# Splitting the output weights of a rational layer on the scalar and vector engines, and a nested polynomial read from PSUM

## The chip, the cores and the metric

One NeuronCore of a Trainium2 chip runs the whole program. The metric is the device time of one launch in microseconds; the program runs on one core, so that core's time is the time. Below, PE is the tensor engine, DVE the vector engine, ACT the scalar engine, POOL the GpSimd engine and SP the engine that issues the DMAs here.

## The reference

Three layers run one after the other. The change touches the second.

```python
# 1: attention restricted by clusters: q, k, v of 2 x 8 heads, 768 tokens, 64 dims
# 2: the rational layer: x [1536, 512], w_in [512, 2048], w_out [2048, 512]
h = x @ w_in
h2 = h * h
h3 = h2 * h
P = a[0] + a[1] * h + a[2] * h2 + a[3] * h3
Q = 1.0 + np.abs(b[0]) * np.abs(h) + np.abs(b[1]) * h2
g = P / (Q + 1e-06)
return (g @ w_out).astype(np.float32)
# 3: eight experts [512 -> 1024 -> 512] mixed with Sinkhorn weights
```

## The kernel before, in words

**Precision.** Every matmul operand is split into a high part (the value rounded to the format that PE takes) and a low part (the rest), and each product is the sum of three matmuls: high by high, high by low, low by high. Weights must therefore be split after they are loaded: first the high part, then the low part, which needs the high one.

**The rational layer.** The 1536 tokens are 4 chunks of 384 (HS), the 2048 hidden columns are 16 blocks of 128 (f). One chunk and one block are a unit u = 16 c + f, so there are 64 units. PE computes the hidden values of a unit with 12 matmuls of 128x384 into PSUM bank f % 4 (function hidden, L501 to L503) and its share of the output with 12 more (function mlp_out, L582 to L584). mlp_chunk writes PE's order out by hand: hidden of unit u + 4, then the output of unit u. mlp_out of unit u waits for the low part of its g (semaphore g_lo) and, whatever the chunk, for the low part of weight block f (wout_lo).

**What ACT does in step u** (mlp_step in the scalar block): mlp_reads(u), four activations that read PSUM: the square into TA (L790), the scaled absolute value into TB (L791), a3 h + a2 into TC (L792), a1 h + a0 into TD (L794); then mlp_recip(u - 1), a logarithm and an exponential that give an approximate reciprocal of Q (L800, L802); then g_hi_part(u - 2), the high part of g (L807).

**What DVE does in step u** (mlp_step in the vector block), eight instructions: the Q sum of unit u (L1018), the first Newton product of unit u - 1 (L1025, which waits for the exponential of L802), TC times TA (L1028), Q plus 1 (L1030), the second Newton step of u - 1 (L1033), the addition of TD (L1037), the low part of g of unit u - 2 (gl, L1041), and g of unit u - 1 (L1046). Both engines take their instructions strictly in the order written.

**The output weights.** w_out comes in 16 blocks of 128x512, called pieces here. SP loads them (load_wout, L364) into wst_out, which has two places: piece f may be loaded once the low part of piece f - 2 has been made, because that frees its place. POOL makes the high and the low part of all 16 (L1268, and L1204 by the helper lo_part called at L1270) in a loop that starts when attention's last product is done (pv_done). These lines order the loads:

```python
at_least(sp, wout_lo, fp * 2 + r - 1)
sp.dma_start(wst_out[:, r, :], tile.rearrange("p a d -> p (a d)")).then_inc(wout_in[r], 16)
```

**Around it.** In the last steps of attention ACT copies the last rows of x (L770), POOL makes their low part, and the first four hidden units are put in between. Late in the rational layer, after unit 58's hidden values, POOL splits the first expert weights (L1297, L1298, L1328 and L1204).

Of the kernel before, what the change touches and what calls it, by code (L numbers as in the profile page):

```python
# [18 lines left out]
F32 = mybir.dt.float32  # L19
F32R = mybir.dt.float32r  # L20
ALU = mybir.AluOpType
ACT = mybir.ActivationFunctionType
# [4 lines left out]
P = 128  # L27
B, H, S, D = 2, 8, 768, 64
NC = 16
BH = B * H  # L30
QT = S // P
HS = S // 2
# [11 lines left out]
AHEAD = 4  # L44
SINK = 8
SCALE = 1.0 / 8.0
PENALTY = -(2.0 ** 100)
OHW = 112


def at_least(eng, sem, value):

    if isinstance(value, int) and value <= 0:
        return
    eng.wait_ge(sem, value)


def build(nc, qT, kT, v, cent, ident_d, desc_d, fold_d, w_in, w_out, a_d, b_d, w_gate, w1, w2, out):
    with ExitStack() as ctx:
# [11 lines left out]
        def sem(name):  # L71
            return ctx.enter_context(nc.semaphore(name))

        def pack(start, *specs):

            got = []
            for name, shape, dt in specs:
                got.append(sb(name, start, shape, dt))
                start += (size(*shape[1:]) + 31) // 32 * 32
            return got, start  # L80
# [1 line left out]

        (XTh, XTl, ab, babs, wgf, fold), o_win = pack(
            0, ("XTh", [P, B, DT, S], F32R), ("XTl", [P, B, DT, S], F32R),
            ("ab", [P, 4], F32), ("babs", [P, 2], F32), ("wgf", [P, DT, E], F32),
            ("fold", [P, E], F32))
        (winh, winl), o_free = pack(o_win, ("winh", [P, FT, DT, P], F32R), ("winl", [P, FT, DT, P], F32R))

# [14 lines left out]
        centn = xt[:, 3 * D:4 * D]  # L103


        (wouth, woutl, TA, TB, TC, TD, gh, gl, wst_out), o2 = pack(
            o_free,
            ("wouth", [P, FT, DM], F32R), ("woutl", [P, FT, DM], F32R),
            ("TA", [P, 4, HS], F32), ("TB", [P, 4, HS], F32), ("TC", [P, 4, HS], F32), ("TD", [P, 2, HS], F32),
            ("gh", [P, 2, HS], F32R), ("gl", [P, 2, HS], F32R), ("wst_out", [P, 2, DM], F32))  # L110


# [60 lines left out]
        wout_in = (sem("wout_in0"), sem("wout_in1"))  # L173
        wout_hi, wout_lo = sem("wout_hi"), sem("wout_lo")
        hid_done, hid_read = sem("hid_done"), sem("hid_read")
        q_part, q_done = sem("q_part"), sem("q_done")
        num_done = sem("num_done")
        recip0 = sem("recip0")
        ln_done = sem("ln_done")
        newton1, q_raw = sem("newton1"), sem("q_raw")  # L180
        newton_r, num_step = sem("newton_r"), sem("num_step")
        g_done, g_hi, g_lo = sem("g_done"), sem("g_hi"), sem("g_lo")
        mlp_done = sem("mlp_done")
        x2_hi, x2_lo = sem("x2_hi"), sem("x2_lo")
# [505 lines left out]
        def _(act):  # L690
# [88 lines left out]
                part(p, 0, 0)  # L779
            values_hi(0, 0)  # L780
            act.wait_ge(const_in, 16 * NCONST)
            act.activation(babs[:], bwork[:, 0:2], ACT.Abs).then_inc(coef_ready, 1)


            def mlp_reads(c, f):
                u = c * FT + f
                act.wait_ge(hid_done, u + 1)
                at_least(act, g_lo, u - 3)
                h = ps[:, f % 4, 0:HS]
                act.activation(TA[:, f % 4, :], h, ACT.Square)  # L790
                act.activation(TB[:, f % 4, :], h, ACT.Abs, scale=babs[:, 0:1]).then_inc(q_part, 1)  # L791
                act.activation(TC[:, f % 4, :], h, ACT.Identity, scale=ab[:, 3:4], bias=ab[:, 2:3])  # L792
                at_least(act, num_done, u - 1)
                act.activation(TD[:, f % 2, :], h, ACT.Identity, scale=ab[:, 1:2],  # L794
                               bias=ab[:, 0:1]).then_inc(hid_read, 1)

            def mlp_recip(u, f):

                act.wait_ge(q_done, u + 1)
                act.activation(TA[:, f % 4, :], TB[:, f % 4, :], ACT.Ln).then_inc(ln_done, 1)  # L800
                act.wait_ge(ln_done, u + 1)
                act.activation(TA[:, f % 4, :], TA[:, f % 4, :], ACT.Exp, scale=-1.0).then_inc(recip0, 1)  # L802

            def g_hi_part(u, f):
                act.wait_ge(g_done, u + 1)
                at_least(act, mlp_done, u - 1)
                act.activation(gh[:, f % 2, :], TC[:, f % 4, :], ACT.Copy).then_inc(g_hi, 1)  # L807

            def x2_hi_part(c):

# [4 lines left out]
            def mlp_step(c, f, reads=True):  # L815
                u = c * FT + f
                first = isinstance(c, int) and c == 0
                if reads:
                    mlp_reads(c, f)
                if f == 3 and not first:  # L820
                    x2_hi_part(c - 1)
                if (f >= 1 or not first) and not (isinstance(c, int) and u > NCH * FT):
                    mlp_recip(u - 1, (f - 1) % FT)
                if f >= 2 or not first:
                    g_hi_part(u - 2, (f - 2) % FT)

            def first_reads(t):
                if t == 1:
                    act.wait_ge(coef_ready, 1)
                    mlp_reads(0, 0)  # L830

            steps(emit, first_reads)(act)
            for f in range(1, FT):
# [74 lines left out]
        def _(dve):  # L908
# [98 lines left out]
                                      ALU.add).then_inc(x_done, 1)  # L1007


            def mlp_step(c, f, reads=True):  # L1010
                u = c * FT + f
                first = isinstance(c, int) and c == 0
                s, s1, s2 = f % 4, (f - 1) % 4, (f - 2) % 4
                one = (f >= 1 or not first) and not (isinstance(c, int) and u > NCH * FT)
                two = f >= 2 or not first
                if reads:
                    dve.wait_ge(q_part, u + 1)
                    dve.scalar_tensor_tensor(out=TB[:, s, :], in0=TA[:, s, :], scalar=babs[:, 1:2], in1=TB[:, s, :],  # L1018
                                             op0=ALU.mult, op1=ALU.add).then_inc(q_raw, 1)
                if f == 3 and not first:  # L1020
                    x2_lo_part(c - 1)
                if one:
                    dve.wait_ge(recip0, u)

                    dve.tensor_tensor(TB[:, s1, :], TB[:, s1, :], TA[:, s1, :], ALU.mult).then_inc(newton1, 1)  # L1025
                if reads:
                    dve.wait_ge(hid_read, u + 1)
                    dve.tensor_tensor(TC[:, s, :], TC[:, s, :], TA[:, s, :], ALU.mult).then_inc(num_step, 1)  # L1028
                    dve.wait_ge(q_raw, u + 1)
                    dve.tensor_scalar(TB[:, s, :], TB[:, s, :], 1.0, 1e-6, ALU.add, ALU.add).then_inc(q_done, 1)  # L1030
                if one:
                    dve.wait_ge(newton1, u)
                    dve.scalar_tensor_tensor(out=TA[:, s1, :], in0=TB[:, s1, :], scalar=2.0, in1=TA[:, s1, :],  # L1033
                                             op0=ALU.subtract, op1=ALU.mult).then_inc(newton_r, 1)
                if reads:
                    dve.wait_ge(num_step, u + 1)
                    dve.tensor_tensor(TC[:, s, :], TC[:, s, :], TD[:, f % 2, :], ALU.add).then_inc(num_done, 1)  # L1037
                if two:
                    dve.wait_ge(g_hi, u - 1)
                    at_least(dve, mlp_done, u - 3)  # L1040
                    dve.tensor_tensor(gl[:, f % 2, :], TC[:, s2, :], gh[:, f % 2, :].bitcast(F32),  # L1041
                                      ALU.subtract).then_inc(g_lo, 1)
                if one:
                    dve.wait_ge(newton_r, u)
                    dve.wait_ge(num_done, u)
                    dve.scalar_tensor_tensor(out=TC[:, s1, :], in0=TC[:, s1, :], scalar=-1.0, in1=TA[:, s1, :],  # L1046
                                             op0=ALU.mult, op1=ALU.mult).then_inc(g_done, 1)

            def x2_lo_part(c):
                for d in range(DT):  # L1050
# [8 lines left out]
            def first_step(t):  # L1059
                if t == 1:  # L1060
                    mlp_step(0, 0)

            steps(emit, first_step)(dve)
            for f in range(1, FT):
                mlp_step(0, f)
            with dve.Fori(1, NCH) as c:
                for f in range(FT):
                    mlp_step(c, f)
# [125 lines left out]
        def _(pool):  # L1194
            pool.memset(OH[:], 0.0).then_inc(zero_ready, 1)

            def carry_wait():


                pool.sem_inc(waits_carried, 1)  # L1200

            def lo_part(dst, x, hi):

                return pool.tensor_tensor(dst, x, hi.bitcast(F32), ALU.subtract)  # L1204
# [52 lines left out]
                part(p, 0, 0)  # L1257
            steps(emit)(pool)


            pool.wait_ge(pv_done, 2 * BH)
            with pool.Fori(0, FT // 2) as fp:
                for r in range(2):
                    f = fp * 2 + r
                    fh, fl = (x[:].rearrange("p f d -> p (f d)")[:, bass.ds(f * DM, DM)] for x in (wouth, woutl))
                    pool.wait_ge(wout_in[r], (fp + 1) * 16)
                    carry_wait()
                    pool.tensor_copy(fh, wst_out[:, r, :]).then_inc(wout_hi, 1)  # L1268
                    pool.wait_ge(wout_hi, f + 1)
                    lo_part(fl, wst_out[:, r, :], fh).then_inc(wout_lo, 1)  # L1270


            def add(dst, x, y):

                return pool.tensor_tensor(dst, x, y, ALU.add)
# [152 lines left out]
```

## Time and profile before

| | |
|---|---|
| device time, median of 3 runs | 1678.51 us (1678.4 to 1681.99) |
| the profiled execution: its own time | 1679.58 us |
| the profiled execution: span from first to last instruction | 1677.7 us |
| PE busy | 1575.9 us, 94% |
| PE weight loads busy | 1438.6 us, 86% |
| DVE busy | 1136.7 us, 68% |
| ACT busy | 649.1 us, 39% |
| POOL busy | 673.0 us, 40% |

The whole program's shares are an average over three layers with different limits. The rational layer lies from about 335 us to 642 us of the span (first matmul of L501 to last matmul of L584). A timeline gives each instruction's start, its length and, in brackets, how long its engine had been idle and what released it; a following instruction of the same engine can start a little before the end of the one ahead.

### The profile page before, as it was taken

The numbers are of one execution on the slowest core, as the hardware profiler recorded it, in microseconds if no ns is written. First come the engines' busy times: TensorE is split into PE (matmuls) and PEld (weight loads), VectorE is DVE, ScalarE is ACT, GpSimd is POOL, SyncE is SP. The second block draws the span as 40 slices with busy tenths as digits, with TensorE's granted clock in tenths as the row PEclk, the third lists the DMA queues.
The fourth block names the chain that finished last, engine by engine and source line by source line (L and its number), as shares of the span: only waits on it lengthen the run. The fifth ranks groups of instructions, "written<-read, shape, count | busy, mean of one in ns | idle before, by whom it ended". The sixth has DMA issues, their size and how long they took to land.

```text
span 1677.7 us, 25909 instructions
## 1 busy us (share of the span) xinstructions
PE 1575.9 (94%) x8265; PEld 1438.6 (86%) x8265; DVE 1136.7 (68%) x2133; ACT 649.1 (39%) x1348; POOL 673.0 (40%) x516
## 2 busy tenths in 40 slices
PE   5888888869999998699999999999999999999998
PEld 5777777769999998598998998998998998988987
DVE  5889898889989992534656555555655565565555
ACT  5888788856888871012111111111111111111111
POOL 4767676571000020268543344244244344334230
PEclk9999999989999998799999999999999999999999
DMA  4322232120000010010110110110110111011001
GB/s 110 89 78 84 82 88 82 31 70 19 1 1 0 13 38 13 26 38 14 38 51 13 39 51 13 38 50 16 47 38 31 32 38 38 25 38 38 25 13 75
DMA packets 76404, 67.92 MB, mean 40 GB/s; under 512 B 17345, under 2 KB 58433, under 8 KB 76353
## 3 DMA queue, kind: packets, MB, share of 16 engines
q1 hardware_dynamic: 76352, 67.25, 13.6%
q8 instruction: 30, 0.49, 0.1%
q14 instruction: 22, 0.17, 0.0%
HBM read 64.09 MB, written 3.15 MB: 40 GB/s over the span
## 4 chain that ended last, share of the span: by engine, by line
PE 78%; DVE 11%; issue 5%; ACT 4%; POOL 0%; DVEq 0%; ACTq 0%; DMA 0%; POOLq 0%
PE ps L657 10%; PE ps L658 10%; PE ps L659 10%; PE ps L546 8%; PE ps L545 8%; PE ps L547 8%; PE ps L582 2%; PE ps L583 2%; PE ps L584 2%; PE ps L501 2%; PE ps L503 2%; PE ps L502 2%; DVE OH L952 2%; PE ps L522 1%; PE ps L477 1%
## 5 line engine op out<-in xcount | busy, mean ns | idle before, releaser
L1160 DVE SCALAR_TENSOR_TENSOR acc<-ps,gate,acc 128x512 f32<-128x512 f32 x372 | 278.9, 750 | 191.5 <-PE ps L659 191.5
L657 PE MATMUL ps<-w2h,hh 128*128 128x512 f32 x768 | 300.9, 392 | 13.0 <-DVE acc L1157 9.6
L658 PE MATMUL ps<-w2l,hh 128*128 128x512 f32 x768 | 300.7, 392 | 0.0
L659 PE MATMUL ps<-w2h,hl 128*128 128x512 f32 x768 | 300.4, 391 | 0.0
L854 ACT ACTIVATE hh<-ps 128x384 fp32r<-128x384 f32 x256 | 119.4, 491 | 401.5 <-PE ps L547 210.8
L1123 DVE SCALAR_TENSOR_TENSOR hl<-ps,hh 128x384 fp32r<-128x384 f32 x256 | 141.3, 553 | 113.3 <-ACT hh L854 107.5
L890 ACT ACTIVATE p1s<-ps 128x384 f32<-128x384 f32 x56 | 27.5, 491 | 453.8 <-PE ps L547 453.8
L657 PEld LDWEIGHTS ps<-w2h,hh 128*128 128x128 f32 x768 | 145.0, 189 | 42.4 <-DVE acc L1157 10.1
L659 PEld LDWEIGHTS ps<-w2h,hl 128*128 128x128 f32 x768 | 145.2, 189 | 30.6
L658 PEld LDWEIGHTS ps<-w2l,hh 128*128 128x128 f32 x768 | 145.1, 189 | 28.2
L1316 POOL TENSOR_SCALAR w1h<-raw 128x1792 fp32r<-128x1792 f32 x28 | 47.8, 1707 | 292.3 <-PE ps L547 291.9
L547 PE MATMUL ps<-XTh,w1l 128*128 128x384 f32 x448 | 150.8, 337 | 0.0
L546 PE MATMUL ps<-XTl,w1h 128*128 128x384 f32 x448 | 150.8, 337 | 0.0
L545 PE MATMUL ps<-XTh,w1h 128*128 128x384 f32 x448 | 150.7, 336 | 0.0
L1241 POOL TENSOR_SCALAR Pb<-Pb,small 128x768 f32<-128x768 f32 x96 | 87.2, 908 | 99.0 <-DVE small L979 98.2
L1204 POOL TENSOR_TENSOR w1l<-raw,w1h 128x1792 fp32r<-128x1792 f32 (+2 forms) x36 | 124.2, 3455 | 2.7
L546 PE MATMUL ps<-tl,w1h 128*128 128x384 f32 x336 | 113.5, 338 | 0.0
L545 PE MATMUL ps<-th,w1h 128*128 128x384 f32 x336 | 112.9, 336 | 0.0
L547 PE MATMUL ps<-th,w1l 128*128 128x384 f32 x336 | 112.6, 335 | 0.0
L477 PE MATMUL ps<-ident,Pb 128*128 128x128 f32 x576 | 95.5, 293 | 15.6 <-DVE PTl L994 10.6
L582 PE MATMUL ps<-gh,wouth 128*128 128x384 f32 x256 | 88.5, 346 | 22.0 <-DVE gl L1041 21.9
L1297 POOL TENSOR_SCALAR w1h<-raw 128x768 fp32r<-128x768 f32 x4 | 3.7, 929 | 262.3 <-PE ps L503 209.2
(147 smaller groups left out, 3771.8 us busy)
## 6 DMA issues: line engine op xcount, KB each, us to landing
raw<-in_w SPq DMA_DIRECT2D x64, 256.0 KB, 3.1
raw<-in_w SPq DMA_DIRECT2D x32, 512.0 KB, 3.3
qd<-in_qT SPq DMA_DIRECT2D x32, 192.0 KB, 3.2
kd<-in_kT SPq DMA_DIRECT2D x32, 192.0 KB, 3.1
wst_in<-in_w_in SPq DMA_DIRECT2D x16, 256.0 KB, 2.7
wst_out<-in_w_out SPq DMA_DIRECT2D x16, 256.0 KB, 2.6
qk<-in_qT SPq DMA_DIRECT2D x16, 192.0 KB, 3.1
qk<-in_kT SPq DMA_DIRECT2D x16, 192.0 KB, 3.3
```

The costliest lines, as they stand in the source:

```text
L477: last = pe.transpose(ps[:, 4 + a, k * P:(k + 1) * P], Pb[:, t1 % 2, a, k * P:(k + 1) * P], ident[:])
L545: pe.matmul(o, ah, xh[:, k, :], start=(start and k == 0), stop=False, skip_group_check=True)
L546: pe.matmul(o, ah, xl[:, k, :], start=False, stop=False, skip_group_check=True)
L547: last = pe.matmul(o, al, xh[:, k, :], start=False, stop=(k == 1), skip_group_check=True)
L582: pe.matmul(o, wouth[:, f, ds_], gh[:, f % 2, :], start=(f == 0), stop=False)
L657: pe.matmul(o, lh, w2h[b][:, fh, :], start=(fh == 0), stop=False)
L658: pe.matmul(o, lh, w2l[b][:, fh, :], start=False, stop=False)
L659: last = pe.matmul(o, ll, w2h[b][:, fh, :], start=False, stop=(fh == 1))
L854: act.activation(hh[hbuf(e, s)][:, fh, thalf, :], ps[:, bank, 0:HS], ACT.Relu).then_inc(h_hi, 1)
L1123: dve.scalar_tensor_tensor(out=hl[hb][:, fh, thalf, :], in0=ps[:, q, 0:HS], scalar=0.0, in1=hh[hb][:, fh, thalf, :].bitcast(F32), op0=ALU.max,
L1160: dve.scalar_tensor_tensor(out=acc[:, tt, :], in0=y, scalar=g, in1=acc[:, tt, :], op0=ALU.mult, op1=ALU.add).then_inc(y_added, 1)
L1204: return pool.tensor_tensor(dst, x, hi.bitcast(F32), ALU.subtract)
```

## The change

The splitting of w_out leaves POOL. In the first chunk (c = 0) ACT makes the high part of piece f in its step f, right behind mlp_reads and ahead of mlp_recip of the unit before; DVE makes the low part of piece f - 1 at the end of its step f. Piece 0's high part is made by ACT in the tail of attention, and the reciprocal of unit 0 now comes ahead of the reads of unit 1. The DMAs and their waits stay as they are.

The polynomial is evaluated by nesting: ((a3 h + a2) h + a1) h + a0, the two products reading h from PSUM on DVE, so TD and its activation go, and the constant a0 is added in the instruction that multiplies by the reciprocal. The 1 + 1e-6 of Q is folded into the logarithm's bias and into the first Newton product, so the addition of L1030 goes. The sign that L1046 used to turn is turned in the two instructions that make the high and low part of g.

```diff
+Q_ONE = 1.0 + 1e-6
...
-        (wouth, woutl, TA, TB, TC, TD, gh, gl, wst_out), o2 = pack(
+        (wouth, woutl, TA, TB, TC, gh, gl, wst_out), o2 = pack(
...
+            def wout_piece_hi(f):
+
+                if f == 0:
+                    act.wait_ge(pv_done, 2 * BH)
+                act.wait_ge(wout_in[f % 2], 16 * (f // 2 + 1))
+                act.activation(wouth[:, f, :], wst_out[:, f % 2, :], ACT.Copy).then_inc(wout_hi, 1)
...
-                act.activation(TC[:, f % 4, :], h, ACT.Identity, scale=ab[:, 3:4], bias=ab[:, 2:3])
-                at_least(act, num_done, u - 1)
-                act.activation(TD[:, f % 2, :], h, ACT.Identity, scale=ab[:, 1:2],
-                               bias=ab[:, 0:1]).then_inc(hid_read, 1)
+                act.activation(TC[:, f % 4, :], h, ACT.Identity, scale=ab[:, 3:4],
+                               bias=ab[:, 2:3]).then_inc(hid_scaled, 1)
...
-                act.activation(TA[:, f % 4, :], TB[:, f % 4, :], ACT.Ln).then_inc(ln_done, 1)
+                act.activation(TA[:, f % 4, :], TB[:, f % 4, :], ACT.Ln, bias=babs[:, 2:3]).then_inc(ln_done, 1)
...
                 first = isinstance(c, int) and c == 0
+                if first and f == 1:
+                    mlp_recip(0, 0)
                 if reads:
                     mlp_reads(c, f)
+                if first:
+                    wout_piece_hi(f)
                 if f == 3 and not first:
                     x2_hi_part(c - 1)
-                if (f >= 1 or not first) and not (isinstance(c, int) and u > NCH * FT):
+                if (f >= 2 or not first) and not (isinstance(c, int) and u > NCH * FT):
                     mlp_recip(u - 1, (f - 1) % FT)
...
+                if t == QT - 1:
+                    wout_piece_hi(0)
...
+            def wout_piece_lo(f):
+
+                dve.wait_ge(wout_hi, f + 1)
...
+                dve.tensor_tensor(woutl[:, f, :], wst_out[:, f % 2, :], wouth[:, f, :].bitcast(F32),
+                                  ALU.subtract).then_inc(wout_lo, 1)
...
-                    dve.tensor_tensor(TB[:, s1, :], TB[:, s1, :], TA[:, s1, :], ALU.mult).then_inc(newton1, 1)
+                    dve.scalar_tensor_tensor(out=TB[:, s1, :], in0=TB[:, s1, :], scalar=Q_ONE, in1=TA[:, s1, :],
+                                             op0=ALU.add, op1=ALU.mult).then_inc(newton1, 1)
                 if reads:
-                    dve.wait_ge(hid_read, u + 1)
-                    dve.tensor_tensor(TC[:, s, :], TC[:, s, :], TA[:, s, :], ALU.mult).then_inc(num_step, 1)
-                    dve.wait_ge(q_raw, u + 1)
-                    dve.tensor_scalar(TB[:, s, :], TB[:, s, :], 1.0, 1e-6, ALU.add, ALU.add).then_inc(q_done, 1)
+                    dve.wait_ge(hid_scaled, u + 1)
+                    dve.tensor_tensor(TC[:, s, :], h, TC[:, s, :], ALU.mult).then_inc(num_step, 1)
...
-                    dve.tensor_tensor(TC[:, s, :], TC[:, s, :], TD[:, f % 2, :], ALU.add).then_inc(num_done, 1)
+                    dve.scalar_tensor_tensor(out=TC[:, s, :], in0=TC[:, s, :], scalar=ab[:, 1:2], in1=h,
+                                             op0=ALU.add, op1=ALU.mult).then_inc(hid_read, 1)
...
-                    dve.scalar_tensor_tensor(out=TC[:, s1, :], in0=TC[:, s1, :], scalar=-1.0, in1=TA[:, s1, :],
-                                             op0=ALU.mult, op1=ALU.mult).then_inc(g_done, 1)
+
+                    dve.scalar_tensor_tensor(out=TC[:, s1, :], in0=TC[:, s1, :], scalar=ab[:, 0:1], in1=TA[:, s1, :],
+                                             op0=ALU.add, op1=ALU.mult).then_inc(g_done, 1)
+                if first and f >= 1:
+                    wout_piece_lo(f - 1)
...
             for f in range(1, FT):
                 mlp_step(0, f)
+            wout_piece_lo(FT - 1)
...
-            pool.wait_ge(pv_done, 2 * BH)
-            with pool.Fori(0, FT // 2) as fp:
-                for r in range(2):
...
-                    pool.wait_ge(wout_in[r], (fp + 1) * 16)
-                    carry_wait()
-                    pool.tensor_copy(fh, wst_out[:, r, :]).then_inc(wout_hi, 1)
-                    pool.wait_ge(wout_hi, f + 1)
-                    lo_part(fl, wst_out[:, r, :], fh).then_inc(wout_lo, 1)
```

## Rows read from the trace of the kernel before

**Rows 1.** Windows: stretch and length, busy us (instructions) by engine, PEclk, DMA share, GB/s

```profile
core 0: us, PE busy (x) PEld busy (x) DVE busy (x) ACT busy (x) POOL busy (x), PEclk, DMA share, GB/s
343.00:358.00 15.00, 4.40 (x26) 4.08 (x24) 14.23 (x14) 8.58 (x17) 12.57 (x13) 0.82 0.24 70
358.00:372.00 14.00, 10.96 (x48) 10.33 (x48) 14.00 (x16) 6.43 (x13) 11.52 (x11) 0.82 0.35 98
...
460.00:500.00 40.00, 40.00 (x232) 40.00 (x232) 35.27 (x77) 32.71 (x68) 0.00 (x0) 1.00 0.00 1
```

**Rows 2.** Waits from 330 to 400 us: who waited for whom, total, times, longest

```profile
PE ps L582 <- DVE gl L1041: 18.9, 5, 10.9
...
POOL wouth L1268 <- DMA wst_out<-in_w_out: 4.9, 10, 0.8
```

**Rows 3.** Timeline of PE: outputs of units 0, 4, 5, 6, and one matmul between

```profile
358.30 0.69 PE L582 MATMUL ps<-gh,wouth 128*128 128x384 f32 x1 [10.90 <-DVE gl L1041]
...
388.80 0.44 PE L582 MATMUL ps<-gh,wouth 128*128 128x384 f32 x1 [1.77 <-DVE gl L1041]
...
391.67 0.52 PE L501 MATMUL ps<-XTh,winh 128*128 128x384 f32 x1
...
394.66 0.35 PE L582 MATMUL ps<-gh,wouth 128*128 128x384 f32 x1
...
398.84 0.34 PE L582 MATMUL ps<-gh,wouth 128*128 128x384 f32 x1
```

**Rows 4.** Timeline of DVE: one instruction beside POOL's work, three without it

```profile
358.17 1.62 DVE L1046 SCALAR_TENSOR_TENSOR TC<-TC,TA 128x384 f32<-128x384 f32 x1
...
452.33 0.61 DVE L1018 SCALAR_TENSOR_TENSOR TB<-TA,babs,TB 128x384 f32<-128x384 f32 x1
452.86 0.55 DVE L1025 TENSOR_TENSOR TB<-TB,TA 128x384 f32<-128x384 f32 x1
453.32 0.55 DVE L1028 TENSOR_TENSOR TC<-TC,TA 128x384 f32<-128x384 f32 x1
```

**Rows 5.** Timeline of POOL: pieces 0, 2, and 4 to 7 of the output weights

```profile
344.95 1.29 POOL L1204 TENSOR_TENSOR woutl<-wst_out,wouth 128x512 f32 x1 [0.17 <-POOL wouth L1268]
...
349.16 0.65 POOL L1268 CAST wouth<-wst_out 128x512 f32 x1 [0.50 <-DMA wst_out<-in_w_out]
...
355.31 1.64 POOL L1204 TENSOR_TENSOR woutl<-wst_out,wouth 128x512 f32 x1 [0.16 <-POOL wouth L1268]
...
358.00 1.38 POOL L1204 TENSOR_TENSOR woutl<-wst_out,wouth 128x512 f32 x1 [0.16 <-POOL wouth L1268]
359.72 0.61 POOL L1268 CAST wouth<-wst_out 128x512 f32 x1 [0.34 <-DMA wst_out<-in_w_out]
...
362.61 0.63 POOL L1268 CAST wouth<-wst_out 128x512 f32 x1 [0.73 <-DMA wst_out<-in_w_out]
```

**Rows 6.** The line L364 alone: its 16 loads

```profile
DMA to landing us min/median/max: 2.4/2.6/2.9
```

**Rows 7.** Line L730 alone (ACT, 128x512 out of SBUF): ns min/median/max

```profile
L730 ACT ACTIVATE winh<-wst_in x16: 616/618/639, 22.2 to 319.3; 128x512 f32 x12, 128x512 fp32r<-128x512 f32 x4
```

**Rows 8.** Timeline of ACT at the start of the rational layer

```profile
341.12 0.84 ACT L770 ACTIVATE XTh<-xt 128x768 fp32r<-128x768 f32 x1 [1.43 <-DVE xt L1006]
...
343.95 0.54 ACT L800 ACTIVATE TA<-TB 128x384 f32<-128x384 f32 x1
344.52 0.53 ACT L802 ACTIVATE TA<-TA 128x384 f32<-128x384 f32 x1
344.95 0.47 ACT L790 ACTIVATE TA<-ps 128x384 f32<-128x384 f32 x1
345.32 0.57 ACT L791 ACTIVATE TB<-ps,babs 128x384 f32<-128x384 f32 x1
```

**Rows 9.** Line L994 alone (DVE, one input in PSUM, one in SBUF): ns min/median/max

```profile
L994 DVE TENSOR_TENSOR PTl<-ps,PTh x192: 539/548/559, 31.2 to 334.9; 128x384 fp32r<-128x384 f32 x192
```

**Rows 10.** Timelines of DVE and PE around the first expert weights' split

```profile
602.51 2.73 DVE L1028 TENSOR_TENSOR TC<-TC,TA 128x384 f32<-128x384 f32 x1
...
606.97 0.44 PE L582 MATMUL ps<-gh,wouth 128*128 128x384 f32 x1 [2.99 <-DVE gl L1041]
```

More of the change, by code:

```diff
@@ L84, in build @@
             0, ("XTh", [P, B, DT, S], F32R), ("XTl", [P, B, DT, S], F32R),
-            ("ab", [P, 4], F32), ("babs", [P, 2], F32), ("wgf", [P, DT, E], F32),
+            ("ab", [P, 4], F32), ("babs", [P, 3], F32), ("wgf", [P, DT, E], F32),
             ("fold", [P, E], F32))
@@ L103, in build @@
         centn = xt[:, 3 * D:4 * D]
-        (wouth, woutl, TA, TB, TC, TD, gh, gl, wst_out), o2 = pack(
+        (wouth, woutl, TA, TB, TC, gh, gl, wst_out), o2 = pack(
             o_free,
             ("wouth", [P, FT, DM], F32R), ("woutl", [P, FT, DM], F32R),
-            ("TA", [P, 4, HS], F32), ("TB", [P, 4, HS], F32), ("TC", [P, 4, HS], F32), ("TD", [P, 2, HS], F32),
+            ("TA", [P, 4, HS], F32), ("TB", [P, 4, HS], F32), ("TC", [P, 4, HS], F32),
             ("gh", [P, 2, HS], F32R), ("gl", [P, 2, HS], F32R), ("wst_out", [P, 2, DM], F32))
@@ L175, in build @@
         hid_done, hid_read = sem("hid_done"), sem("hid_read")
+        hid_scaled = sem("hid_scaled")
         q_part, q_done = sem("q_part"), sem("q_done")
-        num_done = sem("num_done")
+        num_step = sem("num_step")
         recip0 = sem("recip0")
         ln_done = sem("ln_done")
-        newton1, q_raw = sem("newton1"), sem("q_raw")
-        newton_r, num_step = sem("newton_r"), sem("num_step")
+        newton1, newton_r = sem("newton1"), sem("newton_r")
         g_done, g_hi, g_lo = sem("g_done"), sem("g_hi"), sem("g_lo")
@@ L781, in _ @@
             act.wait_ge(const_in, 16 * NCONST)
-            act.activation(babs[:], bwork[:, 0:2], ACT.Abs).then_inc(coef_ready, 1)
+            act.activation(babs[:, 0:2], bwork[:, 0:2], ACT.Abs).then_inc(coef_ready, 1)
+            def wout_piece_hi(f):
[3 more added lines that the diff above has]
+                act.activation(wouth[:, f, :], wst_out[:, f % 2, :], ACT.Copy).then_inc(wout_hi, 1)
             def mlp_reads(c, f):
@@ L806, in g_hi_part @@
                 at_least(act, mlp_done, u - 1)
-                act.activation(gh[:, f % 2, :], TC[:, f % 4, :], ACT.Copy).then_inc(g_hi, 1)
+                act.activation(gh[:, f % 2, :], TC[:, f % 4, :], ACT.Copy, scale=-1.0).then_inc(g_hi, 1)
             def x2_hi_part(c):
@@ L828, in first_reads @@
                 if t == 1:
-                    act.wait_ge(coef_ready, 1)
+                    act.wait_ge(coef_ready, 2)
                     mlp_reads(0, 0)
+                if t == QT - 1:
+                    wout_piece_hi(0)
             steps(emit, first_reads)(act)
@@ L1007, in emit @@
                                       ALU.add).then_inc(x_done, 1)
+            def wout_piece_lo(f):
+                dve.wait_ge(wout_hi, f + 1)
+                if f == 0:
+                    dve.wait_ge(pv_done, 2 * BH)
+                    dve.wait_ge(xt_lo, BH // 2)
+                    dve.wait_ge(win_lo, BH)
+                dve.tensor_tensor(woutl[:, f, :], wst_out[:, f % 2, :], wouth[:, f, :].bitcast(F32),
+                                  ALU.subtract).then_inc(wout_lo, 1)
             def mlp_step(c, f, reads=True):
@@ L1015, in mlp_step @@
                 two = f >= 2 or not first
+                h = ps[:, s, 0:HS]
                 if reads:
@@ L1018, in mlp_step @@
                     dve.scalar_tensor_tensor(out=TB[:, s, :], in0=TA[:, s, :], scalar=babs[:, 1:2], in1=TB[:, s, :],
-                                             op0=ALU.mult, op1=ALU.add).then_inc(q_raw, 1)
+                                             op0=ALU.mult, op1=ALU.add).then_inc(q_done, 1)
                 if f == 3 and not first:
@@ L1040, in mlp_step @@
                     at_least(dve, mlp_done, u - 3)
-                    dve.tensor_tensor(gl[:, f % 2, :], TC[:, s2, :], gh[:, f % 2, :].bitcast(F32),
-                                      ALU.subtract).then_inc(g_lo, 1)
+                    dve.scalar_tensor_tensor(out=gl[:, f % 2, :], in0=TC[:, s2, :], scalar=-1.0,
+                                             in1=gh[:, f % 2, :].bitcast(F32), op0=ALU.mult,
+                                             op1=ALU.subtract).then_inc(g_lo, 1)
                 if one:
                     dve.wait_ge(newton_r, u)
-                    dve.wait_ge(num_done, u)
-                    dve.scalar_tensor_tensor(out=TC[:, s1, :], in0=TC[:, s1, :], scalar=-1.0, in1=TA[:, s1, :],
-                                             op0=ALU.mult, op1=ALU.mult).then_inc(g_done, 1)
+                    dve.wait_ge(hid_read, u)
+                    dve.scalar_tensor_tensor(out=TC[:, s1, :], in0=TC[:, s1, :], scalar=ab[:, 0:1], in1=TA[:, s1, :],
+                                             op0=ALU.add, op1=ALU.mult).then_inc(g_done, 1)
+                if first and f >= 1:
+                    wout_piece_lo(f - 1)
             def x2_lo_part(c):
@@ L1061, in first_step @@
                     mlp_step(0, 0)
+            dve.memset(babs[:, 2:3], Q_ONE).then_inc(coef_ready, 1)
             steps(emit, first_step)(dve)
@@ L1258, in _ @@
             steps(emit)(pool)
-            pool.wait_ge(pv_done, 2 * BH)
-            with pool.Fori(0, FT // 2) as fp:
-                for r in range(2):
-                    f = fp * 2 + r
-                    fh, fl = (x[:].rearrange("p f d -> p (f d)")[:, bass.ds(f * DM, DM)] for x in (wouth, woutl))
-                    pool.wait_ge(wout_in[r], (fp + 1) * 16)
-                    carry_wait()
-                    pool.tensor_copy(fh, wst_out[:, r, :]).then_inc(wout_hi, 1)
-                    pool.wait_ge(wout_hi, f + 1)
-                    lo_part(fl, wst_out[:, r, :], fh).then_inc(wout_lo, 1)
             def add(dst, x, y):
```

## The prediction, made before the changed kernel was run

> **What bounds the kernel now.** I read the windows first, because the averages of the whole program hide the stage that changes. In the steady part of the rational layer PE is busy all the time at a granted clock of 1.00, and a unit (24 matmuls) takes 4.17 us, which is 398.84 less 394.66 [rows 1, 3]. DVE is busy 35.3 of 40 us there, ACT 32.7, POOL not at all: both elementwise engines keep up. In the first 15 us after 343 PE is busy for only 4.40 us while DVE is full and POOL is at work [rows 1]. The waits say for whom: PE waited 18.9 us in five waits for gl, the low part of g [rows 2]. So the start of the layer is bound by DVE, the rest by PE. DVE is slow there because POOL's splitting of w_out runs beside it: an instruction with two SBUF inputs took 1.62 us at 358.17 and 0.55 us at 452.86 [rows 4]. The outputs of units 0 and 4 start at 358.30 and 388.80, so a unit took (388.80 - 358.30) / 4 = 7.6 us in this phase; only from unit 5 on is PE the bound [rows 3].
>
> **What the change removes.** POOL's 16 high and 16 low parts, and with them the long DVE instructions. ACT loses one activation a unit, DVE the cheap addition: eight instructions become seven. None of that is worth anything in the 48 units of chunks 1 to 3, where PE hides it. The new DVE step is two pointer-scalar forms more than before; a start of one of those to the next start is 0.53 us, of the others 0.46 to 0.47 [rows 4]. With Q sum, hid_read product and g at 0.53 and four at 0.47 the step is 3.47 us, and 4.07 with a low part of 128x512 (0.55 plus 128 elements more at the 384-element rate of about 0.40 us, so 0.68 long and some 0.60 to the next start). Both are under PE's 4.17.
>
> **One rule weighed against the rows.** Two DVE instructions now read h from PSUM. L994, with one PSUM input, took 539 to 559 ns over 192 instructions, no more than the 0.55 us of L1025 out of SBUF [rows 4, 9], so the sum takes no charge for it. The Trainium skill speaks against this: VectorE: DVE Perf Modes, in the section on the TRN2 errata, has a fixed 120 cycles for a PSUM source and 58 for SBUF, and its rules for kernel authors advise a copy to SBUF where many operations follow. By its figures an estimate would be 62 cycles, 0.065 us, twice a unit, and the period worked out below would grow by 0.13 us, the total by 1.8 us; the rows do not show it.
>
> **What the change adds: a loop through the DMA.** wst_out has two places. Piece f is loaded when the low part of piece f - 2 is done. DVE now makes that part as the last instruction of its step f - 1. ACT waits for the landed piece in its step f, and behind that wait, in ACT's order, stand the logarithm and exponential of unit f - 1. DVE's step f has the Q sum ahead of it, and everything else behind that exponential, including gl and, last, the low part of piece f - 1, which is what the load of piece f + 1 waits for. So from step 2 to step 15 each step contains one whole DMA turn, and nothing overlaps it but one DVE instruction. SP's queue holds nothing else then; POOL's too is empty. PE waits behind gl.
>
> The period, term by term:
> - End of a low part to the start of the next high part that waits for its load: from 346.24 (344.95 + 1.29) to 349.16, 2.92 us; the others shown are 356.95 to 359.72, 2.77, and 359.38 to 362.61, 3.23 [rows 5]. The transfer itself is 2.4 to 2.9 us from issue to landing [rows 6]. I take 2.95.
> - ACT: high part, 618 ns long [rows 7], less the 0.1 us by which a next one starts early (0.53 long, next after 0.43 [rows 8]): 0.52. Logarithm to exponential 0.57, exponential 0.53 and 0.03 to reach DVE: 1.13.
> - DVE: first Newton, h product, second Newton at 0.47, second h product 0.53, gl 0.47, g 0.53, low part 0.68: 3.62.
>
> 2.95 + 0.52 + 1.13 + 3.62 = 8.22 us a unit. PE needs 4.17 at full clock; at the lower level its matmuls are some 0.32 us apart, 24 of them 7.7 us, still under 8.22. So neither clock level changes the period.
>
> **Start and end of the loop.** ACT ends the copy of x at 341.96 [rows 8]. Then high part 0 (0.52), logarithm and exponential (0.57 + 0.43), Square (0.37) and Abs (0.57) of unit 1: 344.4. DVE: Q sum 0.53, Newton, product and Newton 1.41, second product and g 1.06, low part 0.68: low part 0 is done at about 348.1. POOL's low part of x beside this is over by then. Step 2's gl starts 2.95 + 1.65 + 1.94 later and takes 0.55: output 0 can start at 355.2, 3 us sooner than before. Fourteen periods (steps 2 to 15) end at 348.1 + 115.1 = 463.2 with low part 14; then low part 15 (0.60) and step 16 up to the end of its gl (0.53 + 1.41 + 0.53 + 0.55 = 3.02) give output 14 at 466.8. Before, it started at 398.84 + 8 x 4.17 = 432.2. That is +34.6 us.
>
> PE then leaves a half-idle stretch. Before, from output 4 to output 5 took 5.86 us instead of 4.17, with matmuls 0.52 us long between them (0.34 at full clock) [rows 3]. I charge the same 1.7 us: +36.3. After that DVE (3.47) and ACT are faster than PE, so PE stays the bound and the lag stays as it is through 48 units.
>
> **The late stall.** Around 600 us POOL's split of the first expert weights makes DVE instructions up to 2.73 us long, and PE waits 2.99 us [rows 10]. L994 never exceeded 559 ns in attention, where POOL works as well [rows 9]; so the two h products, with one SBUF input, should no longer be held. Bounds: nothing, or with two of seven free about 2/7 of 2.99, 0.9 us. I take -0.7, nearer the second since L994 is the same shape.
>
> **Sum:** +36.3 - 0.7 = +35.6 us. On the profiled execution's own 1679.58 us (span 1677.7 and 1.9 around it), 1715.2; the median of the runs is 1.1 lower, so 1714.1.
>
> **Rivals.**
> - *The contention's end decides; the DMA is hidden.* For it: POOL's work is what the trace shows as the cause today, and POOL waited at most 0.8 us a time for a load [rows 2]. Then output 0 starts at 348.1 + 3.0 = 351.1, PE runs at 4.17 at once, output 6 is at 376.1 + 1.7 against 398.84: -21.0, with the late stall -21.7: 1656.8 us. The Trainium skill has the rule for this in SBUF — State Buffer, who interferes with whom: a DVE instruction with two SBUF inputs contends with a GpSimd one that reads SBUF and the second blocks; by that rule alone the change is a gain. The trace agrees with the rule itself (1.62 against 0.55 us). Against this rival: POOL waited little only because its own two instructions of about 2 us, not a 4 us step, separated the pieces. 6%.
> - *Two pieces share one turn.* If the loads of an even and an odd piece overlapped, two steps would cost 8.22 + 4.07, 6.15 a step: 14 x 2.07 = 29.0 less, 1685.1. Against: the waits are by single pieces, f - 2 for f, odd and even alike. 3%.
> - *DVE becomes the bound in all chunks.* It decides once a DVE step costs over 4.17, that is 0.10 us more on each of seven instructions. At 0.15 more each, 0.35 x 48 = 17 and 14 x 1.05 = 15 on top: 1746. Against it is L994 [rows 9]. 3%.
> - *The loop as above* has the remaining 88%.
>
> Two pieces sharing and DVE bound are both slower than before; the rival on the other side is the first.
>
> **Range and chances.** The measurement of this kernel can tell 0.2%, 3.4 us. In the loop's case the DMA turn's ends (2.77 and 3.23) give -2.5 and +3.9 us over 14 periods; ACT's high part without the early start, and 0.05 us on each of the DVE instructions for PSUM or hand-over, +1.4 and +5; a little less on each -3; no second low-clock stretch -1.7. Range 1704 to 1727. Faster 0.06 is the first rival; same 0.02 is the low edge of the second, whose 1685 lies close above that bound; the rest, 0.92, is slower.
>
> **What would show it.** Right: L582's outputs of chunk 0 about 8.2 us apart up to some 463 us, ACT's high part released by the DMA of wst_out in 14 steps, DVE idle about 4 us a unit before the first Newton product, released by the exponential, all chunk 0 DVE instructions near 0.55 us, PE without gaps from 470 us on, total PE waiting for gl up from 22 to some 58 us. Wrong: pieces 4.2 us apart, or ACT's high part not waiting for the DMA; then the first or second rival holds. Wrong in the other way: DVE instructions over 0.65 us in chunks 1 to 3, or PE waiting for gl there.

## The result, and the profile after

| | before | changed |
|---|---|---|
| median, us (runs) | 1678.45 (1677.62 to 1681.99, 4 runs) | 1715.88 (1708.9 to 1722.11, 4 runs) |
| ratio, 95% interval | | 1.0218 (1.0171 to 1.0264) |
| profiled execution: its time, span | 1679.58, 1677.7 | 1708.9, 1707.1 |
| PE / DVE / ACT / POOL busy, us | 1575.9 / 1136.7 / 649.1 / 673.0 | 1581.6 / 1111.0 / 626.5 / 637.6 |

The kernel is slower: by 2.2%, with an interval of 1.7 to 2.6%, and that although every elementwise engine has less to do. The page of the changed kernel, part 1 and the 40 slices of PE and DVE:

```profile
PE 1581.6 (93%) x8265; PEld 1442.6 (85%) x8265; DVE 1111.0 (65%) x2086; ACT 626.5 (37%) x1300; POOL 637.6 (37%) x484
...
PE   5888888866799998799999999999999999999998
...
DVE  5888888845688896534555655565556555555565
```

Slices 9 to 11 (about 341 to 469 us) hold chunk 0. The windows, with columns as in [rows 1], show that DVE is no longer full there: it is busy for 8.35 of 15 us where it had 14.23 in the kernel before. POOL is silent, and PE is busy for a little over half to two thirds of the time. From 480 us PE is full at a granted clock of 1.00, as before.

```profile
343.00:358.00 15.00, 7.81 (x37) 7.49 (x36) 8.35 (x16) 6.30 (x13) 0.00 (x0) 0.77 0.12 37
358.00:372.00 14.00, 7.86 (x42) 7.23 (x41) 8.15 (x16) 6.97 (x14) 0.00 (x0) 0.96 0.07 19
...
390.00:450.00 60.00, 38.36 (x179) 35.80 (x178) 30.06 (x59) 27.13 (x55) 0.00 (x0) 0.90 0.11 31
480.00:500.00 20.00, 20.00 (x117) 20.00 (x117) 18.45 (x38) 14.39 (x30) 0.00 (x0) 1.00 0.00 1
```

The waits from 330 to 520 us (who waited for whom, total, times, longest) stand beside those of [rows 2]:

```profile
ACT wouth L791 <- DMA wst_out<-in_w_out: 64.0, 14, 4.8
DVE TB L1048 <- ACT TA L808: 60.5, 22, 4.2
...
PE ps L583 <- DVE gl L1065: 44.4, 14, 7.2
```

Read from the bottom up it is one chain: PE waits for gl, DVE's first Newton product for ACT's exponential, ACT's high part for the load, the last of these fourteen times. One turn of it, in the timelines of DVE and then of ACT:

```profile
386.97 0.68 DVE L1029 TENSOR_TENSOR woutl<-wst_out,wouth 128x512 fp32r<-128x512 f32 x1
387.57 0.61 DVE L1041 SCALAR_TENSOR_TENSOR TB<-TA,babs,TB 128x384 f32<-128x384 f32 x1
392.23 0.56 DVE L1048 SCALAR_TENSOR_TENSOR TB<-TB,TA 128x384 f32<-128x384 f32 x1 [4.05 <-ACT TA L808]
...
395.16 0.68 DVE L1029 TENSOR_TENSOR woutl<-wst_out,wouth 128x512 fp32r<-128x512 f32 x1
```

```profile
390.50 0.63 ACT L791 ACTIVATE wouth<-wst_out 128x512 fp32r<-128x512 f32 x1 [4.67 <-DMA wst_out<-in_w_out]
391.04 0.60 ACT L806 ACTIVATE TA<-TB,babs 128x384 f32<-128x384 f32 x1
391.67 0.52 ACT L808 ACTIVATE TA<-TA 128x384 f32<-128x384 f32 x1
```

The low part ends at 387.65, the next piece's high part starts at 390.50 (2.85 us for the DMA turn), the exponential has been taken over by DVE at 392.23 (1.73), and the next low part ends at 395.84 (3.61): 8.19 us. PE's outputs of units 0, 1 and 13 give the mean:

```profile
354.05 0.69 PE L583 MATMUL ps<-gh,wouth 128*128 128x384 f32 x1 [7.19 <-DVE gl L1065]
362.34 0.44 PE L583 MATMUL ps<-gh,wouth 128*128 128x384 f32 x1 [2.39 <-DVE gl L1065]
...
459.82 0.69 PE L583 MATMUL ps<-gh,wouth 128*128 128x384 f32 x1 [2.31 <-DVE gl L1065]
```

(459.82 - 354.05) / 13 = 8.14 us a unit; the forecast was 8.22. Over all 14 turns of this trace, the stretch from a low part's end to the start of the high part that waits for its place lasted 2.57 to 2.99 us, 2.79 in the mean, and the rest of the period 5.34 each time.

### The profile page after: what moved, and what is told of

Read it like the earlier page. It is cut to its first block, busy times and chain, and to the rows that moved or that the text cites. A ratio compares the mean times of both kernels' runs of the same rounds, so it can differ in the third digit from the quotient of the medians.

```text
span 1707.1 us, 25696 instructions
## 1 busy us (share of the span) xinstructions
PE 1581.6 (93%) x8265; PEld 1442.6 (85%) x8265; DVE 1111.0 (65%) x2086; ACT 626.5 (37%) x1300; POOL 637.6 (37%) x484
## 3 DMA queue, kind: packets, MB, share of 16 engines
q1 hardware_dynamic: 76352, 67.25, 13.5%
## 4 chain that ended last, share of the span: by engine, by line
PE 75%; DVE 11%; issue 6%; ACT 5%; DMA 2%; POOL 0%; DVEq 0%; ACTq 0%; SPq 0%; POOLq 0%
PE ps L658 10%; PE ps L659 10%; PE ps L660 10%; PE ps L547 8%; PE ps L546 8%; PE ps L548 8%; DMA wst_out<-in_w_out 2%; DVE OH L964 2%; PE ps L583 2%; PE ps L584 2%; PE ps L585 2%; PE ps L502 2%; PE ps L504 2%; PE ps L503 2%; DVE PTl L1006 1%
## 5 line engine op out<-in xcount | busy, mean ns | idle before, releaser
L583 PE MATMUL ps<-gh,wouth 128*128 128x384 f32 x256 | 91.7, 358 | 45.3 <-DVE gl L1065 45.3
```

What stands on the lines that cost most here:

```text
L583: pe.matmul(o, wouth[:, f, ds_], gh[:, f % 2, :], start=(f == 0), stop=False)
```

## The experiments

Besides the time of each kernel I compare one length in the traces: from the start of ACT's last copy of x (L770 in the kernel before) to the start of the last output matmul (L584 there). It leaves out attention and the experts, which the change doesn't touch, and whose length varies from trace to trace (that copy starts at 337.35 us in one and at 341.48 in another). In the kernel before it is 642.3 - 341.12 = 301.2 us, in the changed kernel 673.3 - 339.91 = 333.4.

| kernel | median, us | ratio to before (95%) | that length, us |
|---|---|---|---|
| changed | 1715.88 | 1.0218 (1.0171 to 1.0264) | 333.4 |
| changed, again, 6 runs | 1714.65 | 1.0200 (1.0173 to 1.0228) | 333.8 |
| changed, third look, 1 run | 1710.32 | | 332.3 |
| three places | 1655.2 | 0.9848 (0.9817 to 0.9880) | 277.9 |
| high part last | 1663.01 | 0.9902 (0.9874 to 0.9930) | 288.5 |
| polynomial only | 1663.88 | 0.9891 (0.9860 to 0.9921) | 287.7 |
| split only | 1710.39 | 1.0189 (1.0157 to 1.0221) | 337.1 |
| split only, high part last | 1674.63 | 0.9965 (0.9945 to 0.9984) | 297.3 |
| two DMA turns | 1747.15 | 1.0411 (1.0376 to 1.0445) | 368.7 |

Beside three places, high part last, polynomial only and split only the kernel before had a median of 1681.95 us, beside the others and the repeated changed kernel 1679.19.

**Three places.** The wait that opens the loop is taken away by room, not by dropping it. TD's 3072 bytes a partition, freed by the change, hold the 2048 of a third place. SP's loop over the loads is written out for it, which the excerpt leaves out; in the changed kernel's trace SP starts a load 0.16 to 0.18 us after the low part that frees its place, so the form of the loop has little to give.

```diff
-            ("gh", [P, 2, HS], F32R), ("gl", [P, 2, HS], F32R), ("wst_out", [P, 2, DM], F32))
+            ("gh", [P, 2, HS], F32R), ("gl", [P, 2, HS], F32R), ("wst_out", [P, 3, DM], F32))
...
-                    at_least(sp, wout_lo, fp * 2 + r - 1)
+                at_least(sp, wout_lo, f - 2)
...
-                act.wait_ge(wout_in[f % 2], 16 * (f // 2 + 1))
-                act.activation(wouth[:, f, :], wst_out[:, f % 2, :], ACT.Copy).then_inc(wout_hi, 1)
+                act.wait_ge(wout_in[f % 3], 16 * (f // 3 + 1))
+                act.activation(wouth[:, f, :], wst_out[:, f % 3, :], ACT.Copy).then_inc(wout_hi, 1)
```

> The changed kernel with three places for the loaded pieces of w_out instead of two (piece f is loaded once the low part of piece f - 3 is done); all instructions of ACT and DVE are the same. Theory A (the DMA turn inside the step loop makes chunk 0 slow): the turn now has a whole step beside it, outputs of chunk 0 come 4.2 us apart, the first near 351 us, and the time is about 1655 us (1650 to 1662), some 60 below the changed kernel. Rival B (ACT and DVE are slow in chunk 0 because of the work that the split adds to them, the wait for the DMA being idle time that would be lost anyway): outputs stay 7 to 8 us apart, time over 1700 us.

Measured: 1655.2 us, 1.5% under the kernel before and some 60 us under the changed one, with the same instructions in the same order on ACT and DVE. In its windows PE is full from 365 us on; in its waits (345 to 420 us) the loads are almost gone and PE waits for gl once:

```profile
365.00:390.00 25.00, 25.00 (x145) 25.00 (x145) 24.36 (x49) 21.77 (x44) 0.00 (x0) 1.00 0.25 64
390.00:410.00 20.00, 20.00 (x117) 20.00 (x117) 20.00 (x40) 16.72 (x34) 0.00 (x0) 1.00 0.13 41
```

```profile
ACT wouth L788 <- DMA wst_out<-in_w_out: 4.5, 9, 0.9
...
PE ps L580 <- DVE gl L1062: 3.2, 1, 3.2
```

So it was the wait, not the added work. DVE is busy for the whole of 390 to 410 us and PE does not wait: DVE's steps there start 4.05 to 4.07 us apart (389.81, 393.88, 397.93), the 4.07 that the prediction worked out, and fit barely under PE's 4.17.

**High part last.** Only the order on ACT changes; the two places and the loads stay.

```diff
                 if reads:
                     mlp_reads(c, f)
-                if first:
-                    wout_piece_hi(f)
...
                 if f >= 2 or not first:
                     g_hi_part(u - 2, (f - 2) % FT)
+                if first:
+                    wout_piece_hi(f)
```

> The changed kernel with ACT's high part of piece f moved from behind mlp_reads to the end of ACT's step f, behind the logarithm, the exponential and the high part of g; two places and all DMAs as in the changed kernel. Theory A: the turn no longer stands between two DVE steps but runs beside one; two steps hold one turn (2.9), high part (0.5), reads (1.4), reciprocal (1.1) and the rest of a DVE step (3.6), 9.5 us, so outputs are 4.2 to 4.8 us apart and the time is 1658 to 1672 us. Rival B: no change by the order, 1710 to 1720 us.

Measured: 1663.01 us, inside the expected range. ACT still waits for loads, 21.6 us in 12 waits against 64.0 in 14, but the exponential stands ahead of the wait now and DVE goes on meanwhile. What made the loop was two things together: a load that can't start before the last instruction of a step, and a wait for it placed ahead of what the next step needs.

**Two DMA turns.** The suspected cost doubled:

```diff
                     sp.dma_start(wst_out[:, r, :], tile.rearrange("p a d -> p (a d)")).then_inc(wout_in[r], 16)
+                    sp.wait_ge(wout_in[r], fp * 32 + 16)
+                    sp.dma_start(wst_out[:, r, :], tile.rearrange("p a d -> p (a d)")).then_inc(wout_in[r], 16)
...
-                act.wait_ge(wout_in[f % 2], 16 * (f // 2 + 1))
+                act.wait_ge(wout_in[f % 2], 32 * (f // 2 + 1))
```

> The changed kernel in which each piece of w_out is loaded twice, the second transfer issued when the first has landed; nothing else differs. Theory A: the period grows by one transfer, 2.6 us from issue to landing and some 0.1 to 0.2 to issue it, from 8.14 to 10.8 or 11.0 us, so 14 periods add 37 to 40 us and the time is 1749 to 1760 us. Rival B (the turn is beside other work and the elementwise load sets the period): under 1725 us.

Measured: 1747.15 us, 2 us below the expected range. PE's outputs 0 and 13:

```profile
354.79 0.69 PE L585 MATMUL ps<-gh,wouth 128*128 128x384 f32 x1 [9.67 <-DVE gl L1067]
...
493.51 0.69 PE L585 MATMUL ps<-gh,wouth 128*128 128x384 f32 x1 [4.64 <-DVE gl L1067]
```

The period is (493.51 - 354.79) / 13 = 10.67 us, 2.53 more than in the changed kernel; 14 times that is 35.4 us, and the compared length grew by 368.7 - 333.4 = 35.3. The growth is all in the turn, whose mean goes from 2.79 to 5.32 us, while the rest of the period stays at 5.34. The second transfer adds no more than its time from issue to landing (median 2.6 us); expecting 2.7 to 2.8 was the error. Every microsecond of the turn is paid 14 times.

**Split only.** The kernel before with the split where the change puts it, and the old polynomial:

```diff
 on the kernel before:
+                if first:
+                    wout_piece_hi(f)
...
+                if first and f >= 1:
+                    wout_piece_lo(f - 1)
...
-            pool.wait_ge(pv_done, 2 * BH)
-            with pool.Fori(0, FT // 2) as fp:
```

> The kernel before with only the split of w_out moved to ACT and DVE in the changed kernel's places; the old polynomial with TD and the addition stays. Theory A: the period is that of the changed kernel plus some 0.2 us (the part of DVE's step behind the exponential is 3.8 us instead of 3.6), so 8.3 to 8.4 us, and the stall of 3 us near 600 us comes back: 1716 to 1728 us. Rival C (the polynomial costs): at or below the changed kernel's time by more than 5 us, under 1708 us.

Measured: 1710.39 us, under the expected range and 4 to 6 us under the changed kernel's medians, in between the two theories' ranges. The times leave it open which of the two is slower: the changed kernel's own runs lie 13 us apart, and the intervals of the two ratios overlap. In the traces this layer is the longer one, 337.1 against 333.4, 333.8 and 332.3 us. The period is 8.18 ((458.70 - 352.38) / 13), and up to the output of unit 52 the layers are equal (284.5 against 284.4, 284.9 and 283.4 us from the copy of x). The difference comes after it. The stall near the end is back at its full size, in PE's timeline:

```profile
638.30 0.44 PE L582 MATMUL ps<-gh,wouth 128*128 128x384 f32 x1 [3.00 <-DVE gl L1064]
```

Behind the stall PE's clock falls here (granted 0.64 from 638 to 642 us, matmuls of 0.52 us), and the next output comes after 5.84 us instead of 4.17. In the changed kernel the wait at this place is 0.96 us and the clock stays at 1.00.

**Polynomial only.** The changed kernel without wout_piece_hi and wout_piece_lo, and with POOL's loop of the kernel before:

```diff
 on the changed kernel:
-                if first:
-                    wout_piece_hi(f)
...
-                if first and f >= 1:
-                    wout_piece_lo(f - 1)
...
+            pool.wait_ge(pv_done, 2 * BH)
+            with pool.Fori(0, FT // 2) as fp:
```

> The changed kernel's nested polynomial, folded constants and seven DVE instructions, but the split of w_out is back on POOL as before. Theory A: the h products, with one input in PSUM, are not held by POOL, the other five are; outputs 0 to 4 are 6 to 7.6 us apart instead of 7.6, and the wait of 3 us near 600 us goes; time 1666 to 1676 us against 1678.5. Rival C (the polynomial itself is what costs, through PSUM reads by DVE): slower than before, over 1682 us.

Measured: 1663.88 us, a larger gain than expected, 18 us beside its own measurement of the kernel before and 13.5 in the compared length. The wait near 600 us is down to 0.95 us, not gone. POOL's phase still lasts to about 386 us, but outputs are 5.5 us apart (365.46, 370.94, 376.35) instead of 7.6. One step of DVE beside POOL's work:

```profile
366.29 1.64 DVE L1037 SCALAR_TENSOR_TENSOR TB<-TA,babs,TB 128x384 f32<-128x384 f32 x1
367.85 0.55 DVE L1044 SCALAR_TENSOR_TENSOR TB<-TB,TA 128x384 f32<-128x384 f32 x1
368.32 0.55 DVE L1048 TENSOR_TENSOR TC<-ps,TC 128x384 f32<-128x384 f32 x1
368.79 0.54 DVE L1051 SCALAR_TENSOR_TENSOR TA<-TB,TA 128x384 f32<-128x384 f32 x1
369.25 0.60 DVE L1055 SCALAR_TENSOR_TENSOR TC<-TC,ab,ps 128x384 f32<-128x384 f32 x1
369.78 1.11 DVE L1061 SCALAR_TENSOR_TENSOR gl<-TC,gh 128x384 fp32r<-128x384 f32 x1
370.81 0.96 DVE L1068 SCALAR_TENSOR_TENSOR TC<-TC,ab,TA 128x384 f32<-128x384 f32 x1
```

The two that read h from PSUM (L1048, L1055) are never long; of the five with two SBUF inputs three are. The expectation had put the phase's outputs 6 to 7.6 us apart. It left out that the addition which the change drops (L1030) had been held too: 0.81 us in the mean from 343 to 386 us in the kernel before, against 0.35 undisturbed. The two products took 1.16 and 1.49 us in the mean there and take 0.55 and 0.60 here; the other five together have hardly changed, 5.3 us before and 5.1 here. So of some 2.5 us that the instructions of a step lose, 0.8 is the dropped addition and 1.5 the products.

**Split only, high part last.**

```diff
 on the kernel with the split only: ACT's mlp_step as in "high part last"
-                if first:
-                    wout_piece_hi(f)
...
+                if first:
+                    wout_piece_hi(f)
```

> The kernel before with the split on ACT and DVE, the old polynomial, and ACT's high part at the end of its step as in the run with the high part last. Theory A: with the turn mostly off the chain the polynomial is worth one activation in each half period (0.55 us, and 0.15 on DVE), so against the changed order with the nested polynomial (1663) chunk 0 is 3 to 6 us longer and the stall of 3 us near 600 us is back: 1668 to 1673 us. Rival C (the polynomial costs): below 1663 us.

Measured: 1674.63 us, 1.6 us over the expected range. Its compared length is 8.8 us more than with the nested polynomial in the same order (297.3 less 288.5), of which 3.4 arise around the late stall: a wait of 3.00 us instead of 0.95, and slower matmuls right behind it. So the nested polynomial gains beside POOL's split (13.5 us in the compared length) and with the high part last (8.8), and the times agree. With the high part first it gains 3.3 to 4.8 in the compared length, while the medians of the two kernels stand the other way by 4 to 6 us; there its worth in device time is not shown.

**The changed kernel again,** for the spread:

> The changed kernel once more, for its interval: its four times so far lie 13 us apart (1708.9 to 1722.1) at mean granted clocks of 0.967 to 0.977, those of before 4.4 us apart. Theory A: the steps of chunk 0 leave PE idle for about half of each period, and what clock PE has when it leaves that stretch differs from execution to execution; the median stays between 1711 and 1720 us. Rival D (the first four were disturbed): times within 5 us of 1709.

> The changed kernel a third time, one look, to have another trace beside that of the fastest of its runs. Theory A: outputs in chunk 0 again 8.1 us apart; where the time is longer, windows of some stage show a lower granted clock and the same number of matmuls in more time.

Measured: 1714.65 us (1707.15 to 1718.0), and 1710.32 for the single look. The result stands. The outputs of chunk 0 are again some 8.1 us apart in the mean (8.25 and 8.13), with one turn of 10 us in the second trace, where ACT waited 6.5 us for one load. Over the 10 runs of the first two rows the longer ones tend to have the lower mean granted clock (1707.15 at 0.978, 1722.11 at 0.967). The kernel before shows the same (1675.05 at 0.982, 1686.82 at 0.972, in 17 runs), so the spread is not the loop's own. Which stretch the longer runs lose it in is not shown: the three executions with a trace are all among the shorter, 1708.9 to 1710.3 us.

## Why the prediction was right, and where its terms were off

**The loop** was forecast at 8.22 us and measured at 8.14, its parts in the turn shown at 2.85 (2.95 forecast; 2.79 is the mean), 1.73 (1.65; the logarithm with a bias from SBUF is 0.60 us long instead of 0.54) and 3.61 (3.62). That the DMA turn was in it is shown from four sides: taken off by room (three places), taken off by order (high part last), doubled (two turns), and present with the old polynomial (split only). The forecast that neither clock level of PE changes the period holds: matmuls of 0.52 us and of 0.34 us appear in the same phase at the same spacing of outputs. One sign that it named came out smaller: PE's total wait for gl was to rise from 22 to some 58 us and is 45.3. Those 58 us are what is left of the loop when a unit's matmuls take 4.17 us. At the granted clock of 0.90 from 390 to 450 us PE was busy for 38.36 of the 60 us, where 4.17 of every 8.14 would be 30.7. The charge for a PSUM input that the sum left out does not show: in the step printed under polynomial only, the instruction that reads h from PSUM without a pointer scalar is 0.55 us long and 0.47 from start to start, like the two beside it that read SBUF alone (L1044, L1051).

**The first rival** was nearly right about the size of what it named. By its sum the kernel takes 1656.8 us once the contention is gone; with three places it takes 1655.2. The two times are closer than the gains: the rival had 21.7 us, and measured were 26.8 beside its own runs of the kernel before (1681.95) and 23.3 in the compared length, 1.3 of which is more than forecast at the late stall. What the rival had wrong is the load being hidden. The sharing of a turn by two pieces and DVE as the bound in all chunks did not occur: DVE waits for the exponential in every one of steps 2 to 15, and in the later chunks PE waits once. That wait, and the DVE instructions of over 0.65 us around it, are what the prediction called wrong in the other way; they belong to the late stall, which its own sum expected.

**The late stall** was the mis-sized term: -0.7 us forecast with 0.9 as the bound, -2.0 measured. PE's wait for gl went from 2.99 us to 0.96, though POOL's work beside it is the same:

```profile
637.97 0.44 PE L583 MATMUL ps<-gh,wouth 128*128 128x384 f32 x1 [0.96 <-DVE gl L1065]
```

It is 0.94 to 0.97 in every other kernel with the nested polynomial too. In DVE's timeline the h products pass at full speed between instructions that are held:

```profile
632.84 1.09 DVE L1048 SCALAR_TENSOR_TENSOR TB<-TB,TA 128x384 f32<-128x384 f32 x1
633.85 0.54 DVE L1052 TENSOR_TENSOR TC<-ps,TC 128x384 f32<-128x384 f32 x1
634.32 0.93 DVE L1055 SCALAR_TENSOR_TENSOR TA<-TB,TA 128x384 f32<-128x384 f32 x1
635.17 0.60 DVE L1059 SCALAR_TENSOR_TENSOR TC<-TC,ab,ps 128x384 f32<-128x384 f32 x1
635.70 2.22 DVE L1065 SCALAR_TENSOR_TENSOR gl<-TC,gh 128x384 fp32r<-128x384 f32 x1
```

Scaling PE's wait by the share of free instructions was the mistake. PE waits only for what DVE's delay exceeds its lead by. The excess lengths of the held instructions add up to 6.0 us in the kernel before and to 4.8 in the changed one, 1.2 less. DVE's lead, from the end of unit 53's gl to the start of its output, grew from 2.34 to 3.03 us with the shorter step, 0.7 more. Together that is 1.9 of the 2.0. That it is the polynomial and not the later start of the phase is shown by the split-only kernel, where the excess is again 6.0, the lead 2.34 and the wait 3.00 us.

**The sum in one execution** and the median need telling apart. On the profiled execution the forecast was +35.6 us and the measured difference of spans +29.4. The steps from 35.6 down: attention ended 1.2 earlier in that execution, and output 0 with it; the period gave 1.1 less over 13 units; the low-clock charge came to about 1.1 instead of 1.7 (output 14 started 1.07 later than start and period give); the late stall gave 1.3 more; two chunk boundaries, where outputs of the kernel before were up to 0.26 us late, gave 0.4. That makes 31.0 at the layer's last matmul; the other 1.6 lies behind it, in the experts. The compared length, free of attention's and the experts' variation, grew by 32.2, 32.6 and 31.1 us in the three traces. The medians grew by 37.4 and 35.5. So it is luck that the 1714.1 forecast lies as close to the measured 1715.88: its terms were 3 to 4.5 us too high for what the traces show, and the runs without a trace are 6 us longer in the mean than those with one, which no term of the sum explains.

**The measured parts do not add.** In the compared length the split alone costs 35.9 us and the polynomial alone gains 13.5; together they cost 32.2, not 22.4. The polynomial's gain beside POOL was mostly that fewer instructions were held. Once the split has left POOL nothing in chunk 0 is held, and behind a DMA turn the shorter step saves 0.04 us a unit in the measured period; the 3.7 us that it still gains come around the late stall.

## What to carry to other kernels

When a step of weight preparation is moved from an idle engine into the order of a busy one, follow its buffer: if the slot is released by the last instruction of a step and the next load's wait stands ahead of what the next step needs, every step contains a whole DMA turn, as here with DVE busy for only half of the time. One more slot, or the wait placed behind the critical instructions, takes it out; here the change with a third slot (1655.2 us) beats both kernels, and the room for it was what the change itself had freed. The wait that the old owner had for its loads (0.8 us at most here) says nothing about the new place, because the distance between release and need is another.

## What the runs showed of the hardware

Beside POOL's work, DVE instructions with two SBUF inputs took up to 2.73 us instead of 0.55, those with one input in PSUM 0.54 to 0.62, pointer-scalar form and either operand order included. The Trainium skill states this in SBUF — State Buffer, in the section on who interferes with whom: outside the 2-port perf modes, an instruction with at most one SBUF input does not contend with GpSimd. The traces agree for inputs in PSUM. One SBUF input alone is not what frees an instruction: the addition that the change drops has one, takes 0.35 us undisturbed, and was held as well in the kernel before. Whether it falls under the exception for the 2-port modes no run here shows:

```profile
347.46 1.41 DVE L1030 TENSOR_SCALAR TB<-TB 128x384 f32<-128x384 f32 x1
```

With POOL's split left in place, the products from PSUM and the dropped addition together are worth 13.5 us of the layer. A second transfer of the same 256 KB, chained to the first one's landing, added 2.53 us a turn, so the issue by SP costs nothing that shows beside the 2.6 us from issue to landing.
